# A fused attention, gated MLP and routed experts kernel: the norm's first sums and one transposed block's evacuation at other places in the queues

## What is computed

```
scores = q @ k.T / sqrt(64)         # batch 4, 8 heads, 576 positions, head width 64
heads 0-3: causal window of 32; heads 4-7: every 32nd position, causal
attn = softmax(scores masked); x = attn @ v        # -> x: 2304 tokens x 512
rms = sqrt(mean(x*x, axis=-1) + 1e-6)              # the norm
xn = x / rms * rms_g
g = xn @ w_gate;  val = xn @ w_val                 # 512 -> 1536
x = (g * sigmoid(g) * val) @ w_out                 # 1536 -> 512
e = argmax(x @ router + modality_bias[modality_id])
out = softmax(...)[e] * (relu(x @ w1[e]) @ w2[e])   # 8 experts, 512 -> 1024 -> 512
```

## Time and profile before

| what | value |
|---|---|
| three runs | 876.58, 876.9, 878.62 us; median 876.9 us |
| the profiled execution | 878.62 us, of which the span of the trace is 876.9 us |
| PE busy | 860.4 us, 98% of the span |
| DVE, ACT, POOL busy | 521.7, 374.4, 329.5 us |
| mean granted TensorE clock | 0.99 of full speed |

### The profile page before, as it was taken

How to read it: one execution, slowest core, us unless ns; L and a number is a source line. 1 busy time by engine, 2 the same in 40 slices (tenths; PEclk the granted TensorE clock), 3 DMA queues, 4 the chain that set the end, 5 groups by cost and what they waited for, 6 DMA issues and landing times.

```text
span 876.9 us, 15595 instructions
## 1 busy us (share of the span) xinstructions
PE 860.4 (98%) x5233; PEld 737.5 (84%) x5242; DVE 521.7 (60%) x1400; ACT 374.4 (43%) x944; POOL 329.5 (38%) x372
## 2 busy tenths in 40 slices
PE   8999999999999999999999999999999999999995
PEld 5668898888888888899999999998888888888884
DVE  5975555333453335439787773884877447666662
ACT  5966413545454455533221132242456235555440
POOL 3735772345233443247345333170043112122221
PEclk9979999999999999999999999999999999999998
DMA  9964212222114210242131221526275646555520
GB/s 189 288 153 133 61 46 64 73 77 74 55 41 119 64 38 25 73 156 62 48 97 61 61 73 37 213 75 253 96 244 176 227 144 217 204 195 202 180 98 27
DMA packets 77517, 103.40 MB, mean 118 GB/s; under 512 B 38973, under 2 KB 43069, under 8 KB 77312
## 3 DMA queue, kind: packets, MB, share of 16 engines
q1 hardware_dynamic: 73760, 91.16, 33.8%
q0 software_dynamic: 3680, 11.28, 3.7%
HBM read 92.98 MB, written 10.22 MB: 118 GB/s over the span
## 4 chain that ended last, share of the span: by engine, by line
PE 90%; DVE 7%; ACT 1%; issue 1%; POOL 0%; DVEq 0%; POOLq 0%
PE ps L1232 33%; PE ps L1271 15%; PE ps L1789 13%; PE ps L1774 13%; PE ps L1163 3%; PE ps L1192 3%; PE ps L1173 2%; PE ps L1799 2%; PE ps L1139 2%; PE ps L1308 1%; PE ps L649 1%; DVE sm L1509 1%; DVE w_lo L2021 1%; PE ps L1301 1%; DVE h_lo L1589 1%
## 5 line engine op out<-in xcount | busy, mean ns | idle before, releaser
L1024 POOL TENSOR_TENSOR sm<-sm,rinv 72x288 f32<-72x288 f32 (+1 forms) x51 | 45.5, 893 | 177.9 <-DVE rinv L1520 177.8
L1056 POOL TENSOR_TENSOR out_lo<-out_raw,out_hi 128x512 fp32r<-128x512 f32 x72 | 102.6, 1424 | 5.8
L1578 DVE SCALAR_TENSOR_TENSOR h<-h,ps 128x384 f32<-128x384 f32 x72 | 39.8, 553 | 104.5 <-ACT h L1426 103.4
L1054 POOL CAST out_hi<-out_raw 128x512 fp32r<-128x512 f32 x72 | 50.6, 702 | 134.5 <-DMA out_raw<-in_moe_w_out 134.5
L1232 PE MATMUL ps<-x_hi,gate_hi 128*128 128x384 f32 x288 | 100.6, 349 | 0.4 <-DVE h L1578 0.4
L1232 PE MATMUL ps<-x_hi,val_hi 128*128 128x384 f32 x288 | 101.0, 351 | 0.0
L1430 ACT ACTIVATE h_hi<-h 128x384 fp32r<-128x384 f32 x72 | 37.8, 525 | 141.1 <-DVE h L1584 141.0
L1232 PE MATMUL ps<-x_hi,gate_lo 128*128 128x384 f32 x288 | 97.1, 337 | 0.0
L1232 PE MATMUL ps<-x_hi,val_lo 128*128 128x384 f32 x288 | 96.5, 335 | 0.0
L1232 PE MATMUL ps<-x_lo,val_hi 128*128 128x384 f32 x288 | 96.4, 335 | 0.0
L1232 PE MATMUL ps<-x_lo,gate_hi 128*128 128x384 f32 x288 | 93.8, 336 | 0.0
(11 more groups left out here) (277 smaller groups left out, 1952.9 us busy)
## 6 DMA issues: line engine op xcount, KB each, us to landing
w_raw<-in_moe_w SPq DMA_DIRECT2D x72, 512.0 KB, 3.9
out_raw<-in_moe_w_out SPq DMA_DIRECT2D x72, 256.0 KB, 2.6
x_rows<-y_tiles SPq DMA_DIRECT2D x18, 256.0 KB, 2.7
early_w_raw<-in_moe_w SPq DMA_DIRECT2D x8, 512.0 KB, 4.0
gate_raw<-in_moe_w_gate SPq DMA_DIRECT2D x4, 768.0 KB, 8.5
val_raw<-in_moe_w_val SPq DMA_DIRECT2D x4, 768.0 KB, 10.0
qk<-in_q SPq DMA_DIRECT2D x8, 288.0 KB
qk<-in_k SPq DMA_DIRECT2D x8, 288.0 KB
```

Of the source, the lines that this page charges most:

```text
L1024: pool.tensor_tensor(s3, s3, rinv[0:n, i, :].unsqueeze(2).to_broadcast([n, 4, c]), ALU.mult).then_inc(s_no, 1)
L1054: pool.tensor_copy(oh[i][:, :], o_raw[i][:, :]).then_inc(s_oh, 1)
L1056: pool.tensor_tensor(ol[i][:, :], o_raw[i][:, :], oh[i][:, :].bitcast(f32), ALU.subtract).then_inc(s_ol, 1)
L1578: dve.scalar_tensor_tensor(out=hf[n % 2][:, :], in0=hf[n % 2][:, :], scalar=1.0, in1=ps[:, 0, 0:CH], op0=ALU.add, op1=ALU.mult).then_inc(s ...
```

## The change

Two pieces of work get another place in a queue; no instruction is added, removed or altered. On PE, `sum_squares(0)` moves from tick 17, behind `score(17)`, to the end of tick 16, behind that tick's `keep_busy(3)`. On DVE, the copy of block 27 moves from tick 24 to the start of tick 26.

```diff
@@ front_pe
                 for j in SCORE_AT.get(s, []):
                     score(j)
-                if s == SS[0] + 1:
-                    sum_squares(0)
                 for j in TURN_AT.get(s, []):
                     turn_probs(j)
...
                 for c in SS_AT.get(s, []):
-                    if c:
-                        sum_squares(c)
+                    sum_squares(c)
@@ front_dve
                 c, f, sub, half = step_of(s) if s >= EARLY else (0, 0, -1, 0)
+                if s == QK_BY_ACT - 1:
+                    for key in QK_AT.get(s, []):
+                        dst, src = evac_qk(dve, *key)
+                        dve.tensor_copy(dst, src).then_inc(s_qe, 1)
                 if (sub, half) == (1, 0):
...
                 if EARLY <= s < QK_BY_ACT - 1:
-                    for key in QK_AT.get(s, []) + (QK_AT.get(QK_BY_ACT - 1, []) if s == QK_BY_ACT - 3 else []):
+                    for key in QK_AT.get(s, []):
                         dst, src = evac_qk(dve, *key)
                         dve.tensor_copy(dst, src).then_inc(s_qe, 1)
```

## The result

| | before | changed |
|---|---|---|
| median of 5 runs each | 876.58 us (874.81 to 878.62) | 881.49 us (879.48 to 882.39) |
| ratio, 95% interval | 1 | 1.0053 (1.0037 to 1.0069) |
| profiled execution, own time / span | 878.62 / 876.9 us | 880.37 / 878.6 us |

I had forecast 878.2 us and a range up to 880.3; the measured time lies outside it.

What follows compares the result with a forecast made beforehand. PE's matmul queue was taken as the bound, busy 860.4 of 876.9 us. The terms 0.42 + 0.83 = 1.25 us on the 876.9 us median gave 878.15, stated as 878.2 us, range 876.2 to 880.3 us.

Steps and rivals of the forecast that it cites:

- PE's queue passes a delay on: From about 77 us on, PE is one queue of matmuls; earlier losses or gains reach the end almost whole.
- the 0.36 us wait: DVE's wait in tick 24 for PE to turn block 27; moving the copy should remove it.
- PE's wait at block 31: 0.32 us wait before block 31's transpose at 76.85 us, predicted to vanish: -0.32 us.
- Part one: Ticks 16 and 17: sums ahead of the score make PE wait for POOL's square; cost 0.42 us, later roots covered.
- a delay carried into it passes through: In the half-clock stretch, 47.84 to 58.08 us, PE is busy 9.88 of 10.24 us, so it absorbs no delay.
- Part two: Ticks 24 to 27: block 28's transpose waits 1.15 us for block 27's copy; 0.32 us returned, net 0.83 us.
- rival 1: The half-clock stretch past 58.08 us gets longer, adding 1.72 us: 879.9 us; chance 0.22.
- Rival 2: The half-clock stretch gets shorter or falls elsewhere, saving 1.72 us: 876.4 us; chance 0.10.
- Rival 3: DVE's 1.05 us gain hides the 1.15 us wait in tick 27, leaving 0.42 us: 877.3 us; chance 0.12.
- Rival 4: The moved copy has to stand behind POOL's 0.66 us normalise(20): 878.8 us; chance 0.02.

Runs made afterwards that it cites:

- run 10: Not a follow-up run: the words come from "PE had run 10 us at half clock", about the trace of the kernel before.
- the repeat: The changed kernel, unaltered, measured again beside new runs of the kernel before: 880.14 us against 876.66, ratio 1.0043.

## Where the prediction was right and wrong

**Which places, and that PE's queue passes a delay on: right.** Both waits stand where they were said to, on the releasers named, DVE's order shows the 0.36 us wait gone, and PE's wait at block 31 is gone as well. From 80 us to the end nothing made up for them: PE's waits there are those of before (0.7, 0.5 and 0.4 us).

**Part one, 0.42 us: the wait right, its cost open between 0.1 and 0.5 us.** PE's wait for the square was 0.63 us as worked out (44.64 to 45.26), and the roots began at 47.14 us, 2.6 us behind the first sum (the working: 47.9 against 45.26), straight behind `mask_max(17)`, with the spread not waiting. The cost on the whole depends on the price of clock: the rest of the sums moved alone is 0.1 ±0.2 us above before, at equal clock loss it is 0.5 ±0.15, close to the 0.42. What was wrong is the ground given for "a delay carried into it passes through": I had taken the lack of waits between 58 and 77 us from one execution whose PE had been slowed for 10 us. At full clock PE waits there for DVE and ACT anyway; that some of the delay was absorbed in those waits is possible and not shown.

**Part two, 1.15 us of wait, 0.83 net: the mechanism right, the size too small.** In the profile with the same half-clock stretch as before's the wait is 1.03 us. In three others, the changed kernel's among them, it is 2.0 us. The working placed DVE against PE by the trace of before, where PE had run 10 us at half clock and DVE had not. In the changed kernel's profile POOL's cast `gate_hi` ended at 61.7 us, 7.3 us behind PE's first gate matmul; in before the same end was 62.98, only 5.7 us behind. In the mean over runs the copy costs 1.1 ±0.2 us of rest, or 1.4 ±0.15 at equal clock loss, against 0.83. That the sum of both, 1.25 us, agrees with the rest of the changed kernel (1.2 ±0.2) is partly luck: by the split, part one was too high and part two too low, and at equal clock loss the two cost 2.0 us and not 1.25.

**The clock: this is the step that failed.** The sum, 0.42 + 0.83 = 1.25 us, holds nothing for it. It was in the text as rival 1, with 0.22, priced at 1.72 us and tied to one condition, that the four fill matmuls of tick 19 alone don't bring the clock back. Three things were wrong with that.
- It was treated as a case that happens or doesn't. The runs show an addition to the mean, which belonged in the sum: 2.7 ±0.4 us of clock loss, in full 877.0 + 1.2 + 2.7 = 880.9 us, or at 0.71 us each 877.0 + 2.0 + 1.9 = 880.9 us.
- It looked at one place. I named a fall of the clock around the sums, and never asked what a PE wait of one to two microseconds in tick 27 does to it. Filled with matmuls whose result nobody reads, that wait goes with 1.9 us less clock loss.
- Its condition was wrong in place. In the changed kernel's three profiles of the stretch (the first, the repeat and the one with fill at block 28) the clock was back before the first gate product each time; what varied was how long it had been down.

The Trainium skill, TensorE: Matmul & The Clock Gate, section "What's actually happening", says that the slow clock is the default and activity releases it. The fill experiments agree (clock loss 6.0, 4.6 and 3.8 us with none, two and four more fill matmuls), and its remark that the number of slow matmuls differs between runs of one kernel agrees with half-clock stretches at the same place of 3.3 and 6.8 us in two profiles of the changed kernel, and of 10.2 and 3.4 us in two of the copy moved alone.

**The other rivals.** Rival 2, the shorter stretch, did come in the changed kernel's profile (3.25 us instead of 10.24 at the sums) and saved nothing, as the clock fell again at block 28. Rival 3, all of the copy's wait hidden, fell: the copy alone costs 1.1 us of rest. Rival 4 fell: the moved copy took 0.63 us in the changed kernel while POOL's `normalise(20)` ran.

**What stays open.** Why the moved sums alone lose clock: the 0.6 us of idleness, or the longer row of small matmuls between two fills (0.42 us longer by the moved score). The fill in front of them took the loss back, but it stands in for the idleness and cuts the row of thin work at once. And what a microsecond of lost clock costs at each place: the 0.71 is a mean over places, and the parts of the 3.9 us move with it, from 1.2 + 2.7 at a full price to 2.0 + 1.9.

## What to carry to other kernels

A queue that looks full may be full because its engine runs at half clock: before you call a delay passed on or absorbed, ask at which clock the trace was taken, and what the other engines would do to the fast engine. If a change makes PE wait between dense matmuls, or lengthens a row of tiny ones, put the price of half clock behind it into the sum, not among the rivals; and when runs of one kernel spread by more than the effect, split each run's time by its mean granted clock and compare the means of both parts, with the price of lost clock taken from the spread of one kernel's own runs (here 0.7 us for each us, not 1). Fill matmuls in a place where PE would wait can be worth more than they take.

## What the runs showed of the hardware that I had not expected

- A single PE wait of 2.0 us between dense float32 matmuls was followed by half clock in three of three profiles, for 3.3 to 7 us; with a wait of 1.03 us in one profile it was not. In that profile the half-clock stretch at the sums was also the longer one (10.2 us against 3.3 to 6.8), so it isn't shown that the length of the wait alone decides.
- PE shown busy without a gap is no protection: in the changed kernel the clock fell at 609.8 us, behind a row of 24 matmuls of 8 columns that lasted 2.7 us, with PE busy for 3.76 of the 3.76 us ahead of the fall and for 3.40 of 3.40 us at half clock, a clock loss of about 1.7 us. The profile of before has the same row and no half clock behind it; six of the twelve of the experiments have it.

```profile
606.38 2.74 PE L1819 MATMUL ps<-rw,yT_c 128*128 128x8 f32 x24
```

- Half clock explains most of the spread of this kernel's times: in the two experiments with the sums alone the fastest run (875.51 us) had a mean clock of 0.997 and the slowest (884.42 us) 0.984, which is 11.5 us of clock loss for 8.9 us of time. A straight line on clock loss accounts for 90% of the variance of before's 98 times.
